# Who begins the weight loads of the first layer: SyncE or ScalarE

## The chip, the cores and the metric

The kernel runs on one core of a Trainium2 chip. The metric is the device time of one launch in microseconds (us), as the median of some runs. The core has five engines with a queue of instructions each: TensorE (PE in the rows; PEld is its weight load), VectorE (DVE), ScalarE (ACT), GpSimd (POOL) and SyncE (SP). SyncE computes nothing and only begins transfers. The transfers themselves are carried out by 16 DMA engines, whichever engine began them. Engines wait for one another through semaphores.

## What is computed

The reference, cut to what matters (4 batches, 8 heads, 576 queries and keys, head size 64; then two dense blocks over 2304 tokens, 512 features wide with 2048 hidden features):

```python
def _attn_ref(q, k, v, tau):
    scale = 1.0 / np.sqrt(q.shape[-1])
    scores = scale * np.matmul(q, k.transpose(0, 1, 3, 2))
    thresh = np.max(scores, axis=-1, keepdims=True) - tau
    scores = np.where(scores >= thresh, scores, -1000000000.0)
    scores = scores - np.max(scores, axis=-1, keepdims=True)
    attn = np.exp(scores)
    attn = attn / (np.sum(attn, axis=-1, keepdims=True) + 1e-09)
    return np.matmul(attn, v)
# x = the heads side by side, (2304, 512)
# first layer:  g = s * relu(x @ w_in)**2 + b;   x = g @ w_out
# second layer: h = x @ w_in2;  g = h * sigmoid(1.702 * h);  out = g @ w_out2
```

## The kernel before

**Beats.** Attention is cut into 160 score tiles of up to 128 queries, two to a *beat*; there are 85 beats. The tiles belong to 32 groups of one pair of heads: *long* groups (384 queries, three beats) and *short* ones (192 queries, two beats). In each beat TensorE makes two tiles of scores, VectorE takes their row extremes (L1045) and masks them (L1071), ScalarE takes the exponent between the two (L1269), GpSimd norms the rows (L1554), and VectorE turns the tile in blocks of 32x32 into `blocks` (L1085), which has room for two groups.

**The moves.** The turned blocks still lie in the wrong partitions. SyncE puts them in place with transfers `prob_t <- blocks` (`move_quad`, L639 to L651, four transfers each). For a long group eight of them come in one beat (its first half) and eight in the next (its second half); for a short one eight and four. They wait until the whole group is turned and until the earlier readers of that half of `prob_t` are done. Two things wait for them: `context_of` on TensorE (L777 to L809), which multiplies `prob_t` with the values, and VectorE's first turn of the group after next (L1081 to L1084), which writes over `blocks`.

**The first layer beside it.** From beat 15 (`MLP_FROM`) on, each beat also holds one *step* s = beat - 15 of the first layer: one slab of 128 hidden features for a tile of 384 tokens. There are 96 steps; steps 0 to 69 run beside attention (beats 15 to 84), steps 70 to 95 alone. TensorE computes `hidden(s)` (L831) and `output(s - 3)` (L850); ScalarE makes the gate (L1325), the high part of the gated values (L1332), and the high parts of both weight slabs (`slab_in_hi` L1311, `slab_out_hi` L1318); GpSimd makes the low parts of the weights (L1560, L1567), in place, in the memory of `w_raw`. Each float32 product is made of three products of high and low parts.

**The loads.** Load n (512 KB) brings the input slab n and the output slab n - 3 from HBM into slot n mod 5 of `w_raw`. There are 99 loads (0 to 98); the first three and the last three carry only one of the two slabs. Load n waits until `hidden(n - 5)` and, from n = 8, `output(n - 8)` are done, since these read the slot. Loads 0 to 3 are begun by SyncE in beat 1; from beat 15 on SyncE begins load beat - 11, that is, s + 4, in each beat, and loads 74 to 98 in the steps after attention (L713 to L715).

**SyncE's order in a beat** is written by hand and never overtaken: loads of queries, loads of keys, the moves of that beat, the weight load (L687, L688), loads of values (L678 to L694). **ScalarE's order in a beat** (L1425 to L1461): exponents, copies of attention results, `gated_hi(s - 1)`, `slab_out_hi(s - 1)`, splits of queries and keys (L1253, L1259), `gate_of(s)`, `slab_in_hi(s + 2)`. In the beats in which a token tile ends, `gate_of` comes before `slab_out_hi`.

Of the kernel before, what the change touches and what calls it, by code (L numbers as in the profile page):

```python
# [118 lines left out]
def q_load_beat(i):  # L119
    return max(0, q_split_beat(i) - (1 if Q_LOADS[i][0] < LONE_GROUPS else 2))  # L120
# [38 lines left out]
def key_load_beat(e):  # L159
    return max(0, key_free_beat(e), key_split_beat(e) - 2)  # L160
# [15 lines left out]
STEPS = LAYER_TILES * SLABS  # L176
# [4 lines left out]
IN_HI, OUT_HI, LO_RING = 3, 3, 5  # L181
IN_LEAD = 3
# [49 lines left out]
MLP_FROM = 15  # L232
# [34 lines left out]
def riding(beat):  # L267
    return PIECE_OF[beat] if beat in PIECE_OF and rides(PIECE_OF[beat]) else None


def alone(beat):
    return PIECE_OF[beat] if beat in PIECE_OF and not rides(PIECE_OF[beat]) else None
# [42 lines left out]
def tiles_of(beat, lag=0):  # L315
    return range(2 * beat - lag, 2 * beat - lag + 2)
# [41 lines left out]
def build(nc, q, k, v, consts_in, ident_in, slabs, twin_in, twin_out, out):  # L358
    ctx = ExitStack()
    with ctx:  # L360
        def sem(name):
            return ctx.enter_context(nc.semaphore(name))

        def sbuf(stack, name, shape, dt=F32):
            return stack.enter_context(nc.sbuf_tensor(name, shape, dt))
# [48 lines left out]
        w_raw = sbuf(raw, "w_raw", [P, LO_RING, 2, D_MODEL])  # L414
# [83 lines left out]
        w_loaded = [sem(f"w_loaded{n}") for n in range(LO_RING)]  # L498
# [4 lines left out]
        h_ready = sem("h_ready")  # L503
# [4 lines left out]
        y_step_done = sem("y_step_done")  # L508
# [39 lines left out]
        def out_of(ring, n):  # L548

            return ring[:, (n + IN_LEAD) % LO_RING, 1, :]  # L550
# [10 lines left out]
        def h_bank(n):  # L561

            if n < FIRST_PURE:
                return shared
            return (scores[0][:, 1, :], scores[1][:, 0, :], scores[1][:, 1, :])[n % H_RING]
# [50 lines left out]
        def _(sp):  # L616
            def load_q(i):

                if i >= Q_RING:
                    sp.wait_ge(q_lo_ready, i - Q_RING + 1)  # L620
                sp.dma_start(q_raw[:, i % Q_RING, 0:q_width(i)], q[i][:, 0:q_width(i)]).then_inc(q_loaded[i % Q_RING], 16)

            def load_k(e):

                if key_slot(e) >= STORE and key_before(e) is None:
                    sp.wait_ge(context_ready, LONE_PIECES)
                if key_before(e) is not None:
                    sp.wait_ge(scores_ready, key_tiles(key_before(e))[-1] + 1)
                if e >= 2:
                    sp.wait_ge(k_hi_ready, e - 1)  # L630
                sp.dma_start(k_raw[key_slot(e)][:], k[e]).then_inc(k_loaded[e % 2], 16)

            def load_values(i):

                if i >= 2:
                    sp.wait_ge(context_ready, VALUES[i - 2][2] + 1)
                sp.dma_start(v_sb[:, i % 2, :, :, :], v[i]).then_inc(v_loaded[i % 2], 16)
# [15 lines left out]
            def move_quads(w, beat):  # L653
                for a in range(quads_of(w)):
                    if beat == FIRST_BEAT[w] + (4 if is_long(w) else 3) + a // 2:
                        move_quad(w, a)

            def load_weights(n):

                parts = slice(0 if n < STEPS else 1, 1 if n < IN_LEAD else 2)  # L660
                if n >= LO_RING:
                    sp.wait_ge(h_ready, n - LO_RING + 1)
                if n >= LO_RING + IN_LEAD:
                    sp.wait_ge(y_step_done, n - LO_RING - IN_LEAD + 1)
                sp.dma_start(w_raw[:, n % LO_RING, parts, :], slabs[slab_row(n), :, parts, :]
                             ).then_inc(w_loaded[n % LO_RING], 16)
# [11 lines left out]
            for beat in range(BEATS):  # L678
                for i in range(3, len(Q_LOADS)):
                    if q_load_beat(i) == beat:  # L680
                        load_q(i)
                for e in range(2, HEADS):
                    if key_load_beat(e) == beat:
                        load_k(e)
                for w in range(PE_GROUPS, len(GROUPS_OF)):
                    move_quads(w, beat)
                if beat >= MLP_FROM:  # L687
                    load_weights(beat - MLP_FROM + IN_LEAD + 1)  # L688
                if beat == 1:
                    for n in range(IN_LEAD + 1):  # L690
                        load_weights(n)
                for i in range(2, len(VALUES)):
                    if PIECES[VALUES[i - 2][2]][2] == beat:
                        load_values(i)  # L694
# [549 lines left out]
        def _(act_eng):  # L1244
# [16 lines left out]
            def exponent(j):  # L1261

                m, r = rows_of(j), j % STATS
                act_eng.wait_ge(max_ready, j + 1)
                if PROBS <= j < PE_TILES + PROBS:
                    act_eng.wait_ge(rows_pe_turned, j - PROBS + 1)
                elif j >= PROBS:
                    act_eng.wait_ge(turned, j - PROBS - PE_TILES + 1)
                nc.scalar.activation(prob[0:m, j % PROBS, :].rearrange("p (a n) -> p a n", a=2),  # L1269
                                     scores[j % 2][0:m, :, 0:HALF], ACT.Exp,  # L1270
                                     bias=neg_max[0:m, r:r + 1], scale=-1.0).then_inc(exp_ready, 1)

            def context_hi(piece):

                c, start = piece_place(piece)
                act_eng.wait_ge(context_ready, piece + 1)
                if start >= HALF_TOKENS and piece_place(piece - 1)[1] < HALF_TOKENS:
                    act_eng.wait_ge(scores_ready, key_tiles(2 * HEADS_PER_BATCH - 1)[-1] + 1)
                nc.scalar.copy(act_at(act_hi, c, start, piece_size(piece)), piece_bank(piece)
                               ).then_inc(context_hi_ready, 1)  # L1280
# [32 lines left out]
            def slab_out_hi(n):  # L1313

                act_eng.wait_ge(w_loaded[(n + IN_LEAD) % LO_RING], 16 * ((n + IN_LEAD) // LO_RING + 1))
                if n >= OUT_HI:
                    act_eng.wait_ge(y_step_done, n - OUT_HI + 1)
                nc.scalar.copy(wout_hi[n % OUT_HI][:], out_of(w_raw, n)).then_inc(wout_hi_ready, 1)  # L1318

            def gate_of(n):  # L1320

                act_eng.wait_ge(h_ready, n + 1)
                if n >= 2:
                    act_eng.wait_ge(g_lo_ready, n - 1)
                nc.scalar.activation(gate[:, n % 2, :], h_bank(n)[:, 0:TOK], ACT.Relu).then_inc(gate_ready, 1)  # L1325
# [90 lines left out]
            def tile_ends(s):  # L1416
                return s >= OUT_LAG and (s - OUT_LAG) % SLABS == SLABS - 1
# [7 lines left out]
            for beat in range(BEATS):  # L1425
                s = beat - MLP_FROM
                if alone(beat - 1) is not None:
                    context_hi(alone(beat - 1))
                for j in tiles_of(beat):
                    if j < TILES:  # L1430
                        exponent(j)
                    if j % 2 == 0 and 0 <= j - 4 < PE_TILES:
                        copy_tails(j - 4)
                    if j % 2 == 0 and turn_due(s) is not None:
                        x_riding(s)
                if riding(beat) is not None:
                    context_hi(riding(beat))
                for j in tiles_of(beat, 4):
                    if 0 <= j < PE_TILES:
                        copy_main(j)  # L1440
                if tile_ends(s - 1) and s + 1 < STEPS:
                    slab_in_hi(s + 1)
                if s >= 1:
                    gated_hi(s - 1)
                if tile_ends(s):
                    copy_rows(s - OUT_LAG)
                    if s < STEPS:
                        gate_of(s)
                if s >= 1:
                    slab_out_hi(s - 1)  # L1450
                for i in range(2, len(Q_LOADS)):
                    if q_split_beat(i) == beat:
                        split_q(i)
                for e in range(2, HEADS):
                    if key_split_beat(e) == beat:
                        split_k(e)
                if not tile_ends(s):
                    if 0 <= s < STEPS:
                        gate_of(s)
                    if 0 <= s + 2 < STEPS:  # L1460
                        slab_in_hi(s + 2)  # L1461
# [181 lines left out]
def slab_row(n):  # L1643
    return n % SLABS
# [57 lines left out]
```

## Time and profile before

| | us |
|---|---|
| median of 3 runs | 1011.58 (1011.28 to 1013.16) |
| the profiled execution | 1009.4 |
| its span from first to last instruction | 1007.6 |

| engine | busy, us | share of the span |
|---|---|---|
| TensorE, matmul | 993.2 | 99% |
| TensorE, weight load | 895.4 | 89% |
| VectorE | 798.0 | 79% |
| GpSimd | 657.9 | 65% |
| ScalarE | 606.6 | 60% |

The granted TensorE clock is at its full level in all 40 slices of the span. All of the kernel's own transfers stand on one DMA queue, "q1 hardware_dynamic", with 141.34 MB. Times in the trace count from the span's start. Attention ends at about 490 us, the first layer at about 615 us; the rest is the second layer. In the rows, "PE L807" is an instruction of line 807 on TensorE, and "[0.86 <-DMA prob_t<-blocks]" is idle time of the engine just before the instruction, with what ended it. SyncE's instructions ("SPq") are the beginnings of transfers; their duration is the time that the beginning takes on SyncE's queue, and the landing of the data is told apart.

### The profile page before, as it was taken

To read this page: it belongs to the slowest core of one execution; us is meant where nothing else is said; L and a number is where in the kernel's file an instruction comes from. 1 tells how busy PE (TensorE), PEld (TensorE's weight loads), DVE (VectorE), ACT (ScalarE), POOL (GpSimd) and SP (SyncE) were. 2 spreads that over 40 slices of the span, in tenths; PEclk is the share of its full clock that TensorE was granted. 3 is DMA by queue.
4 is the path that set the end of the run, shared out by engine and by line. 5 is a ranking of instruction groups with operands and counts; after the bars stand their busy time and mean duration, and the time that the engine had idled before them with its cause. 6 is when DMAs were issued, how large, how long until landed. Compare 5 with 4: busy or idle time off the path is not lost.

```text
span 1007.6 us, 18212 instructions
## 1 busy us (share of the span) xinstructions
PE 993.2 (99%) x5922; PEld 895.4 (89%) x5922; DVE 798.0 (79%) x1749; ACT 606.6 (60%) x1124; POOL 657.9 (65%) x713
## 2 busy tenths in 40 slices
PE   8999999999999999999999999999999999999998
PEld 7788888888888888888899999998989989899897
DVE  7989999999999999999547766877767776566663
ACT  7877666666676666765555755555546555454443
POOL 6769997778788888886657775454544545445452
PEclk9999999999999999999999999999999999999999
DMA  7236776897977797778733541112122221222212
GB/s 216 73 116 187 209 204 189 218 239 213 228 199 191 204 246 190 209 179 217 211 106 126 185 150 32 63 42 85 44 82 87 102 84 46 81 87 102 84 48 79
DMA packets 97581, 142.50 MB, mean 141 GB/s; under 512 B 10320, under 2 KB 68944, under 8 KB 97488
## 3 DMA queue, kind: packets, MB, share of 16 engines
q1 hardware_dynamic: 97488, 141.34, 48.7%
q8 instruction: 49, 0.80, 0.3%
q14 instruction: 44, 0.36, 0.1%
HBM read 102.96 MB, written 4.72 MB: 107 GB/s over the span
## 4 chain that ended last, share of the span: by engine, by line
PE 85%; DVE 11%; issue 1%; DMA 1%; ACT 1%; POOL 0%; SPq 0%; DVEq 0%; POOLq 0%; ACTq 0%
PE shared L831 12%; PE y_ps L850 11%; PE shared L924 10%; PE y_ps L948 10%; PE scores L948 10%; PE scores L924 8%; PE scores L745 7%; PE scores L807 7%; PE scores L831 5%; PE y_ps L870 5%; DVE scores L1045 4%; DVE prob L1071 3%; PE scores L870 2%; DVE blocks L1085 1%; DMA k_raw<-k 1%
## 5 line engine op out<-in xcount | busy, mean ns | idle before, releaser
L1269 ACT ACTIVATE prob<-scores,neg_max 128x576 f32<-128x576 f32 (+1 forms) x160 | 118.6, 742 | 122.5 <-DVE scores L1045 122.4
L1614 POOL TENSOR_TENSOR a_sum_lo<-a_sum,a_hi 128x256 fp32r<-128x256 f32 x96 | 70.1, 740 | 182.5 <-DVE scores L1167 123.9
L1560 POOL TENSOR_TENSOR w_lo<-w_raw,win_hi 128x512 fp32r<-128x512 f32 x96 | 129.1, 1345 | 22.1 <-ACT win_hi L1311 17.7
L1567 POOL TENSOR_TENSOR w_lo<-w_raw,wout_hi 128x512 fp32r<-128x512 f32 x96 | 126.5, 1318 | 23.4 <-ACT wout_hi L1318 23.4
L1045 DVE TENSOR_SCALAR_CACHE_REDUCE scores<-scores,consts 128x576 f32<-128x576 f32 (+1 forms) x160 | 129.5, 809 | 13.1 <-PE scores L745 11.7
L1554 POOL TENSOR_SCALAR prob<-prob,row_inv 128x576 f32<-128x576 f32 (+1 forms) x160 | 126.8, 805 | 6.1 <-DVE row_inv L1059 5.7
L1071 DVE SCALAR_TENSOR_TENSOR prob<-scores,limit,prob 128x576 f32<-128x576 f32 (+1 forms) x160 | 128.1, 808 | 0.3
L831 PE MATMUL shared<-act_hi,win_hi 128*128 128x384 f32 x280 | 94.8, 339 | 1.1 <-DVE gate L1101 0.9
L831 PE MATMUL shared<-act_hi,w_lo 128*128 128x384 f32 x280 | 94.3, 337 | 0.0
L831 PE MATMUL shared<-act_lo,win_hi 128*128 128x384 f32 x280 | 93.9, 335 | 0.0
L1085 DVE STREAM_TRANSPOSE blocks<-prob 128x576 f32<-128x576 f32 (+1 forms) x128 | 91.4, 751 | 1.9 <-DMA prob_t<-blocks 1.7
L1108 DVE SCALAR_TENSOR_TENSOR g_lo<-gate,consts,g_hi 128x384 fp32r<-128x384 f32 x96 | 92.7, 966 | 0.2 <-ACT g_hi L1332 0.2
L1179 DVE TENSOR_TENSOR g_lo<-gate,g_hi 128x384 fp32r<-128x384 f32 x96 | 62.2, 650 | 33.4 <-ACT g_hi L1403 32.8
L745 PE MATMUL scores<-k_hi,q_hl 128*128 128x288 f32 (+1 forms) x320 | 76.6, 320 | 6.8 <-DVE prob L1071 6.2
L1332 ACT ACTIVATE g_hi<-gate,consts 128x384 fp32r<-128x384 f32 x96 | 59.0, 614 | 38.8 <-PE y_ps L870 27.9
L1395 ACT ACTIVATE gate<-scores 128x384 f32<-128x384 f32 x48 | 23.6, 492 | 94.9 <-DVE scores L1167 94.9
L1403 ACT CAST g_hi<-gate 128x384 fp32r<-128x384 f32 x96 | 49.2, 514 | 49.4 <-DVE gate L1174 40.0
L850 PE MATMUL y_ps<-wout_hi,g_hi 128*128 128x512 f32 x192 | 75.6, 394 | 0.0
L850 PE MATMUL y_ps<-wout_hi,g_lo 128*128 128x512 f32 x192 | 75.5, 393 | 0.0
L807 PE MATMUL scores<-prob_t,v_sb 128*64 128x192 f32 x800 | 73.8, 331 | 1.5 <-DVE prob L1071 0.9
L850 PE MATMUL y_ps<-w_lo,g_hi 128*128 128x512 f32 x192 | 74.9, 390 | 0.0
L1532 POOL TENSOR_TENSOR q_hl<-q_raw,q_hl 128x384 fp32r<-128x384 f32 (+1 forms) x51 | 49.0, 961 | 37.7 <-DVE g_lo L1108 31.2
(157 smaller groups left out, 2956.6 us busy)
## 6 DMA issues: line engine op xcount, KB each, us to landing
w_raw<-slabs SPq DMA_DIRECT2D x93, 512.0 KB, 4.2
a_raw<-twin_in SPq DMA_DIRECT2D x24, 512.0 KB, 4.6
o_raw<-twin_out SPq DMA_DIRECT2D x24, 512.0 KB, 3.6
prob_t<-blocks SPq DMA_DIRECT2D x96, 120.0 KB, 2.8
k_raw<-k SPq DMA_DIRECT2D x32, 288.0 KB, 4.6
prob_t<-blocks SPq DMA_DIRECT2D x96, 96.0 KB, 2.9
v_sb<-v SPq DMA_DIRECT2D x26, 320.0 KB, 4.3
q_raw<-q SPq DMA_DIRECT2D x40, 192.0 KB, 4.4
```

The lines of the kernel that those rows point to most:

```text
L745: mm = nc.tensor.matmul(scores[j % 2][0:m, half, 0:HALF], q_hl[i % Q_RING][:, q0:q0 + m], part[key_slot(e)][:, half * HALF:(half + 1) * HALF],
L807: mm = nc.tensor.matmul(place, v_sb[:, i % 2, side, c, :], rows, start=(c == 0), stop=(c == KEY_CHUNKS - 1))
L831: mm = nc.tensor.matmul(bank[:, 0:TOK], wp[:, w], act_at(xp, c, tile * TOK, TOK), start=(c == 0 and k == 0), stop=(c == DC - 1 and k == 2))
L850: mm = nc.tensor.matmul(y_ps[g][:], gp[:, n % 2, toks], wp[:, :], start=(f == 0 and k == 0), stop=(f == SLABS - 1 and k == 2))
L924: mm = nc.tensor.matmul(twin_bank(x), wp, xp, start=(c == 0 and k == 0), stop=(c == 1 and k == 2))
L948: mm = nc.tensor.matmul(z_bank(tile, g), gp[:, i, toks], wp, start=(e == 0 and i < 2 and k == 0), stop=(e == TWIN_SLABS - 1 and i >= 2 and ...
L1045: nc.vector.tensor_scalar(place, place, scale_c[0:m, :], None, ALU.mult, ALU.min, accum_out=neg_max[0:m, j % STATS:j % STATS + 1]).then_in ...
L1071: nc.vector.scalar_tensor_tensor(out=p, in0=scores[j % 2][0:m, :, 0:HALF], scalar=limit[0:m, r:r + 1], in1=p, op0=ALU.is_le, op1=ALU.mult, ...
L1269: nc.scalar.activation(prob[0:m, j % PROBS, :].rearrange("p (a n) -> p a n", a=2), scores[j % 2][0:m, :, 0:HALF], ACT.Exp, bias=neg_max[0: ...
L1554: nc.gpsimd.tensor_scalar(prob[0:m, j % PROBS, :], prob[0:m, j % PROBS, :], row_inv[0:m, r:r + 1], 1.0, ALU.mult, ALU.mult).then_inc(norme ...
L1560: nc.gpsimd.tensor_tensor(in_of(w_lo, n), in_of(w_raw, n), win_hi[n % IN_HI][:].bitcast(F32), ALU.subtract).then_inc(win_lo_ready, 1)
L1567: nc.gpsimd.tensor_tensor(out_of(w_lo, n), out_of(w_raw, n), wout_hi[n % OUT_HI][:].bitcast(F32), ALU.subtract).then_inc(wout_lo_ready, 1)
```

## The change

ScalarE begins the weight loads 4 to 73 instead of SyncE. In beat 15 + s it begins load s + 4, right behind `slab_out_hi(s - 1)` and ahead of the splits of queries and keys (in beats in which a token tile ends, `gate_of(s)` is already done by then). The waits are the same two semaphores, now waited for on ScalarE's queue. Loads 0 to 3 and 74 to 98 stay with SyncE. Nothing else changes.

```diff
--- before.py
+++ after.py
@@ -684,8 +684,6 @@
                         load_k(e)
                 for w in range(PE_GROUPS, len(GROUPS_OF)):
                     move_quads(w, beat)
-                if beat >= MLP_FROM:
-                    load_weights(beat - MLP_FROM + IN_LEAD + 1)
                 if beat == 1:
                     for n in range(IN_LEAD + 1):
                         load_weights(n)
@@ -1317,6 +1315,16 @@
                     act_eng.wait_ge(y_step_done, n - OUT_HI + 1)
                 nc.scalar.copy(wout_hi[n % OUT_HI][:], out_of(w_raw, n)).then_inc(wout_hi_ready, 1)
 
+            def load_weights(n):
+
+                parts = slice(0 if n < STEPS else 1, 2)
+                if n >= LO_RING:
+                    act_eng.wait_ge(h_ready, n - LO_RING + 1)
+                if n >= LO_RING + IN_LEAD:
+                    act_eng.wait_ge(y_step_done, n - LO_RING - IN_LEAD + 1)
+                nc.scalar.dma_start(w_raw[:, n % LO_RING, parts, :], slabs[slab_row(n), :, parts, :]
+                                    ).then_inc(w_loaded[n % LO_RING], 16)
+
             def gate_of(n):
 
                 act_eng.wait_ge(h_ready, n + 1)
@@ -1448,6 +1456,8 @@
                         gate_of(s)
                 if s >= 1:
                     slab_out_hi(s - 1)
+                if s >= 0:
+                    load_weights(s + IN_LEAD + 1)
                 for i in range(2, len(Q_LOADS)):
                     if q_split_beat(i) == beat:
                         split_q(i)
```

## Rows read from the trace of the kernel before

**Rows 1.** Stretches: length; PE, PEld, DVE, ACT, POOL busy us; clock; DMA share; GB/s.
```profile
66.00:120.00 54.00, 51.63 (x331) 45.29 (x328) 51.45 (x133) 40.01 (x79) 49.97 (x54) 1.00 0.66 194
...
300.00:400.00 100.00, 99.91 (x644) 88.35 (x642) 96.08 (x240) 67.26 (x127) 83.02 (x93) 1.00 0.80 212
```

**Rows 2.** Chain that ended last: start, us, what; 255 to 270.
```profile
255.25 2.10 PE shared L831 x12
...
260.47 2.10 PE shared L831 x12
...
267.74 2.10 PE shared L831 x12
```

**Rows 3.** Timeline of SyncE's queue, 289 to 310: start, us, line, operation.
```profile
289.91 0.53 SPq L665 DMA_DIRECT2D w_raw<-slabs  x1
...
291.93 5.24 SPq L649 DMA_DIRECT2D prob_t<-blocks  x8
297.27 0.53 SPq L665 DMA_DIRECT2D w_raw<-slabs  x1
...
309.56 0.33 SPq L665 DMA_DIRECT2D w_raw<-slabs  x1
```

**Rows 4.** The same queue: one long weight-load issue, two second-half batches.
```profile
243.85 1.46 SPq L665 DMA_DIRECT2D w_raw<-slabs  x1
...
357.30 5.47 SPq L649 DMA_DIRECT2D prob_t<-blocks  x8
...
422.09 5.19 SPq L649 DMA_DIRECT2D prob_t<-blocks  x8
```

**Rows 5.** DMA view, issue to landing: moves at 289.3, 296.8, 362.4, 427.0; load at 297.3.
```profile
prob_t<-blocks SPq DMA_DIRECT2D x1, 96.0 KB, 2.3
...
prob_t<-blocks SPq DMA_DIRECT2D x1, 96.0 KB, 5.6
...
prob_t<-blocks SPq DMA_DIRECT2D x1, 96.0 KB, 4.9
...
prob_t<-blocks SPq DMA_DIRECT2D x1, 96.0 KB, 5.4
...
w_raw<-slabs SPq DMA_DIRECT2D x1, 512.0 KB, 6.9
```

**Rows 6.** Timeline: first readers of the moves on PE, and VectorE's wait.
```profile
165.09 0.51 PE L807 MATMUL scores<-prob_t,v_sb 128*64 128x192 f32 x3 [0.24 <-DMA prob_t<-blocks]
...
302.29 1.44 DVE L1085 STREAM_TRANSPOSE blocks<-prob 128x576 f32<-128x576 f32 x2 [0.86 <-DMA prob_t<-blocks]
...
302.79 0.54 PE L807 MATMUL scores<-prob_t,v_sb 128*64 128x192 f32 x3
...
367.79 0.38 PE L807 MATMUL scores<-prob_t,v_sb 128*64 128x192 f32 x2
...
433.22 0.55 PE L807 MATMUL scores<-prob_t,v_sb 128*64 128x192 f32 x4
```

**Rows 7.** Timeline of ACT and DVE around 295, and a slab's use.
```profile
294.63 0.60 ACT L1318 CAST wout_hi<-w_raw 128x512 fp32r<-128x512 f32 x1
...
295.66 0.47 ACT L1325 ACTIVATE gate<-shared 128x384 f32<-128x384 f32 x1
...
297.52 0.60 DVE L1101 SCALAR_TENSOR_TENSOR gate<-shared,consts,gate 128x384 f32<-128x384 f32 x1
...
310.02 0.61 ACT L1311 CAST win_hi<-w_raw 128x512 fp32r<-128x512 f32 x1
```

**Rows 8.** Timeline of ACT and DVE in beat 16.
```profile
77.51 0.62 ACT L1318 CAST wout_hi<-w_raw 128x512 fp32r<-128x512 f32 x1
78.02 0.51 ACT L1325 ACTIVATE gate<-shared 128x384 f32<-128x384 f32 x1
...
78.67 0.60 DVE L1101 SCALAR_TENSOR_TENSOR gate<-shared,consts,gate 128x384 f32<-128x384 f32 x1
```

**Rows 9.** One microsecond in which mostly loads ran (columns as in Rows 1).
```profile
358.00:359.00 1.00, 1.00 (x8) 1.00 (x7) 0.96 (x4) 0.69 (x2) 1.00 (x2) 1.00 1.00 400
```

## The prediction

> **What bounds the kernel now.** I read the stretches first. Between 300 and 400 us TensorE is busy for 99.91 of 100 us, with VectorE at 96.08 [rows 1]. A busy TensorE says little by itself, since its matmuls overlap, so I looked next at the rhythm in the chain of waits: the first-layer products begin at 255.25, 260.47 and 267.74, so a beat without a context product takes 5.22 us and one with it 7.27 us [rows 2]. These two lengths (7.15 to 7.27, and 0.2 us more where rows are transposed) come back in every beat from 34 to 78, and the chain there passes through TensorE alone. This is a floor that TensorE sets by its own work. The reader is to see that nothing which merely frees another engine can shorten these 45 beats. Only the first part has air: from 66 to 120 us TensorE is idle for 54 - 51.63 = 2.4 us, and VectorE is busy for 51.45 of these 54 [rows 1]; VectorE sets the pace there.
>
> Then I read SyncE's queue, since the change takes work from it. A weight load holds it for 0.53 us behind other transfers, 0.33 us where the queue was quiet [rows 3], and once 1.46 us [rows 4]. A second-half batch of eight moves takes 5.24 us to begin [rows 3]. The DMA view gives the time from beginning to landing: a move at the end of a first-half batch lands after 2.3 us, one at the end of the following second-half batch after 5.6 us [rows 5]. So by the second batch the DMA engines are behind: load 38, values, queries and keys were begun between 289.91 and 291.93 [rows 3] and their bytes still stand ahead of the moves.
>
> **Part 1: the loads themselves.** 70 of 99 loads change hands. Load 39 was begun at 297.27 and took 6.9 us to land, at 304.2 [rows 3, 5]; its first reader comes at 310.02 [rows 7], a margin of 5.8 us, and it is among the smallest of the 70 (the least is 5.5). ScalarE begins load 39 behind the copy at 294.63 [rows 7], 2.6 us earlier; where it comes later than SyncE did, it is by at most 6 us in beats whose margin is over 11. Both waits are already met at that point: the gated values that ScalarE copied just before need `hidden(s - 1)`, and the copy itself waited for `output(s - 4)`. Cost of this part: nothing, covered by those margins.
>
> **Part 2: ScalarE's queue.** 70 beginnings are added. The trace has none on ScalarE, so I bound one from both sides: 0 if it runs beside the copy of 0.60 us ahead of it [rows 7], 0.33 to 0.53 if it takes its time alone as on SyncE [rows 3], 1.46 at worst [rows 4]; below zero is excluded, since work is only added. Queued behind it are the splits, the gate, the next input slab and the next exponent. The nearest to be missed is the gate: at 295.66 + 0.47 = 296.13 it is ready, VectorE takes it at 297.52 [rows 7], so 1.4 us are free there; over the beats from 18 on this slack is 1.1 us or more. An ordinary beginning costs nothing in those beats. In beat 16 it is different: the gate is ready at 78.02 + 0.51 = 78.53 and VectorE starts on it at 78.67 [rows 8], 0.14 us later, in the stretch where VectorE sets the pace. With 0.33 us on the queue, 0.33 - 0.14 = 0.2 us are lost and not won back. I take 0.2 (between 0 and 1.3), by the row of the quiet queue, since SyncE begins nothing else near 78.
>
> The Trainium skill, Perfetto Trace Analysis, "Per-engine timelines", says that a ScalarE instruction is pushed into a wait queue and the sequencer goes on to the next one; a beginning would then run beside the copy and the 0.2 would be 0. No run here shows a transfer begun by ScalarE.
>
> **Part 3: SyncE's queue.** Each beat loses about 0.58 us there (297.27 to the next beginning). What stood behind a load comes that much earlier: values, the next beat's queries, keys and moves. Where does anyone wait for them? TensorE waits once, 0.24 us at 165.09 [rows 6], for the short batch of group 11, which stood right behind a load. Gain: 0.24 us at most, and I take it. VectorE waits three times (the longest 0.86 us, at 302.29 [rows 6]) and the beats around keep their floor length, so that is worth nothing.
>
> **Part 4: the DMA engines.** This is the part that decides. Until now each load stood behind the batch of moves of its beat, in one queue. ScalarE begins it at its copy, and in the beats that end long groups this falls into the second-half batch: load 39 at about 295, into the batch of 291.93 to 297.17 [rows 3, 7]. The moves behind it then share the engines with 512 KB. In a microsecond full of loads they moved 400 GB/s, which is 0.4 MB in a us [rows 9], so the load's 0.512 MB are worth 1.28 us of all engines. The last moves of the batch land later by d. If the engines have no gap, d = 1.28; if the batch, begun 0.58 us earlier, keeps that lead, d = 0.7; if the two queues fill gaps of each other, d = 0, or below it by the 0.58; if the long packets of a load are taken before several short ones of a move, d could reach 2. I take 1.28, by the landing rows: 5.6 against 2.3 us [rows 5] say that the engines are behind, and an earlier beginning buys nothing then.
>
> How late may they be? The last of eight begins at 291.93 + 7/8 x 5.24 = 296.5 and lands at 302.1 (VectorE, waiting for it, starts at 302.29); TensorE's context product starts at 302.79: margin 0.7 us [rows 3, 5, 6]. The same sum at 357.30 gives 362.1 + 4.9 = 367.0 against 367.79, margin 0.8; at 422.09 it gives 426.6 + 5.4 = 432.0 against 433.22, margin 1.2 [rows 4, 5, 6]. There are six such places (second halves of groups 16 to 26, the even ones); the other three have 1.3, 1.4 and 1.6. All other batches have over 2.5 us. TensorE has no slack in these beats, so what goes past a margin lengthens the span. At d = 1.28 this is 0.58 + 0.48 + 0.08 = 1.14 us.
>
> Of the way in which the DMA engines choose between two queues nothing can be seen here, as only one queue is used. The Trainium skill, DMA: Bandwidth & Descriptors, "Queues, rings and completion order", says that each engine takes turns between the queues it has work for, packet by packet; load 39 would then not wait for the moves begun before it, which is the case with d above 0.7. The same page, "Issuing engines are not separate DMA queues", adds that a second issuing engine saves only time on the sequencer.
>
> **The sum.** +1.14 (part 4) + 0.2 (part 2) - 0.24 (part 3) = +1.1 us. The profiled execution would go from 1009.4 to 1010.5 (span 1007.6 to 1008.7). The median of the runs lies 2.2 us above the profiled execution, so the forecast is 1011.58 + 1.1 = 1012.7 us. A measurement of this kernel can tell about 0.2%, 2.0 us, from no change.
>
> **The rivals.** *All is hidden* (d below 0.7): the two queues fill each other's gaps. For it: in the heaviest microseconds the rate is well below 400 GB/s with moves alone. Time: 1011.58 + 0.2 - 0.24 = 1011.5. *The moves come too late* (slower): one mechanism, its place the six second-half batches. From d = 1.45 on the sum of what passes the six margins is over 1.9 us; at d = 2 it is 1.3 + 1.2 + 0.8 + 0.7 + 0.6 + 0.4 = 5.0, so 1016.6. For it: DMA share at or near 1 in that stretch [rows 9] and moves of small packets. Against it: 512 KB are worth only 1.28 at the rate seen. *ScalarE is held* (slower): while SyncE begins eight moves, ScalarE's beginning takes 1.46 us or more, and passes the gate's slack of 1.1 by 0.36. VectorE, at 96%, wins back little of that. In some 12 beats with a batch in the way this is 12 x 0.36 = 4.3, so 1015.9. *SyncE's relief is worth something* (faster): moves, queries and keys come 0.58 us earlier. Its ceiling is TensorE's idle time from 66 to 120 us, 2.4 us [rows 1], and the 0.24 at 165, if all of it hung on SyncE: 1011.6 - 2.6 = 1009.0; but most of these stalls are released by VectorE, not by transfers. That ScalarE begins its loads at a point far from SyncE's and nothing at all changes is part of the first rival.
>
> **Chances.** Forecast (d from 0.7 to 1.45, 1011.5 to 1013.5) 0.45; all hidden 0.17; moves too late 0.22; ScalarE held 0.08; faster by over 2 us 0.08. Hence faster 0.08, within 0.2% 0.62, slower 0.30. For 8 in 10 the range takes in the forecast, the hidden case and most of the slower ones: 1010.8 to 1016.6.
>
> **What would show it.** Part 2: a row of ScalarE's queue for each load, 0.3 to 0.6 us long, and idle time before VectorE's L1101 in beat 16. Part 3: no more wait before the context product near 165. Part 4: landing times of the last moves of the six batches up from 5.6, 4.9 and 5.4 by about 1.3; VectorE's wait at 302 grown from 0.86 towards 2; TensorE's L807 waiting for DMA at two or three places with 1.1 us in all; beats elsewhere still 5.2 and 7.2 us long. The prediction is wrong if the beats between the six places change length, if the landing times do not move, or if anything differs behind attention, where the change touches nothing.

## The result, and the profile after

The changed kernel takes 1012.31 us (median of 18 runs, 1010.30 to 1016.06), the kernel before on the same chip 1009.71 us (18 runs, 1008.58 to 1013.16). The ratio is 1.0026, 95% interval 1.0016 to 1.0037: it is 1.6 to 3.7 us slower, 2.6 us at the median. A second comparison on another occasion (below) gave 1.0012. I had forecast +1.1 us.

The page of the profile after (its span is 1012.2 us, 4.6 us above the 1007.6 us of before):

```profile
span 1012.2 us, 18212 instructions
...
q1 hardware_dynamic: 87408, 104.63, 38.2%
q10 hardware_dynamic: 10080, 36.70, 11.9%
...
PE 79%; DVE 10%; DMA 4%; SPq 4%; issue 2%; ACT 1%; POOL 0%; ACTq 0%; DVEq 0%
...
w_raw<-slabs ACTq DMA_DIRECT2D x70, 512.0 KB, 4.4
```

The 70 loads have gone to a queue of their own, q10, with 36.70 MB, and the chain that ended last now runs through DMA and SyncE's queue for 4% each (before: 1% and 0%). The waits from 66 to 500 us (engine, line, what it waited for: us in total, times, longest) say for what:

```profile
DVE blocks L1083 <- DMA prob_t<-blocks: 10.0, 6, 3.4
PE scores L805 <- DMA prob_t<-blocks: 4.5, 4, 2.2
```

Before, VectorE waited for moves three times [rows 6 has the longest, 0.86 us]; now six times, and TensorE's 4.5 us are nearly the whole growth of the span. These are TensorE's four waits in its timeline (start, length, line, and in brackets the idle time before it and what ended it):

```profile
271.01 1.85 PE L805 MATMUL scores<-prob_t,v_sb 128*64 128x192 f32 x20 [0.85 <-DMA prob_t<-blocks]
305.79 1.85 PE L805 MATMUL scores<-prob_t,v_sb 128*64 128x192 f32 x20 [2.22 <-DMA prob_t<-blocks]
371.96 1.85 PE L805 MATMUL scores<-prob_t,v_sb 128*64 128x192 f32 x20 [1.11 <-DMA prob_t<-blocks]
404.78 1.85 PE L805 MATMUL scores<-prob_t,v_sb 128*64 128x192 f32 x20 [0.34 <-DMA prob_t<-blocks]
```

and these are three of VectorE's six, in its timeline, the largest and the two where TensorE does not wait:

```profile
305.66 1.44 DVE L1083 STREAM_TRANSPOSE blocks<-prob 128x576 f32<-128x576 f32 x2 [3.43 <-DMA prob_t<-blocks]
338.05 1.44 DVE L1083 STREAM_TRANSPOSE blocks<-prob 128x576 f32<-128x576 f32 x2 [0.52 <-DMA prob_t<-blocks]
437.29 1.44 DVE L1083 STREAM_TRANSPOSE blocks<-prob 128x576 f32<-128x576 f32 x2 [0.80 <-DMA prob_t<-blocks]
```

The reader is to see that 271, 305, 338, 371, 404 and 437 are the second halves of groups 16, 18, 20, 22, 24 and 26: the six places of part 4, and no other. I call them the six batches, and the load of the same beat (steps 30, 35, 40, 45, 50 and 55) the load inside; the load of the step before it is the load ahead.

At 290 to 298 the queues of ScalarE and SyncE show how one of them comes about (start, length, line, transfer; compare [rows 3] and [rows 7]):

```profile
290.35 0.33 ACTq L1325 DMA_DIRECT2D w_raw<-slabs  x1
292.16 5.46 SPq L649 DMA_DIRECT2D prob_t<-blocks  x8
293.29 0.74 ACT L1267 ACTIVATE prob<-scores,neg_max 128x576 f32<-128x576 f32 x1 [0.88 <-DVE scores L1043]
293.59 0.34 ACTq L1325 DMA_DIRECT2D w_raw<-slabs  x1
293.93 0.61 ACT L1309 CAST win_hi<-w_raw 128x512 fp32r<-128x512 f32 x1
...
294.95 0.61 ACT L1316 CAST wout_hi<-w_raw 128x512 fp32r<-128x512 f32 x1
```

The load inside is begun at 293.59, while the exponent still runs and 1.36 us ahead of the copy that stands in front of it in the program. In most of the 70 beginnings, this one among them, the load comes about 0.3 us behind the end of TensorE's last product of `output(s - 4)`, for which it has to wait. What the engines then did, one microsecond each from 296, 297, 298 and 299 (DMA queue: packets, MB, time of its packets as a share of 16 engines):

```profile
q1 hardware_dynamic: 272, 0.24, 97.7%
q10 hardware_dynamic: 7, 0.03, 20.5%
...
q10 hardware_dynamic: 31, 0.13, 69.1%
q1 hardware_dynamic: 86, 0.06, 42.7%
...
q10 hardware_dynamic: 49, 0.20, 88.8%
q1 hardware_dynamic: 28, 0.02, 11.9%
...
q10 hardware_dynamic: 46, 0.14, 52.8%
q1 hardware_dynamic: 167, 0.12, 50.9%
```

In the two microseconds ahead of these, from 294 to 296, q10 moved nothing, so for some 2.5 us the load hardly moves a byte. (The load ahead, begun at 290.35, has no packet in q10 before 291 either, so a part of the 2.5 us comes with any load.) Then it has most of the engines for about three microseconds, and the moves in q1 fall from 0.24 MB in a microsecond to 0.02. With the two microseconds behind these (9.4% and 1.7%) q10's packets take 2.4 us of all 16 engines for 0.52 MB. The two moves begun last meanwhile landed late (issues within 296.9 to 297.65; size, median us from issue to landing):

```profile
prob_t<-blocks SPq DMA_DIRECT2D x2, 96.0 KB, 7.9
```

Before, the two begun last took 5.1 us. (For the very last move alone it is 8.5 us here, and 5.6 before [rows 5].)

### The profile page after: what moved, and what is told of

Same layout as the page of the kernel before. It is cut to its first block, busy times and chain, and to the rows that moved or that the text cites. A ratio compares the mean times of both kernels' runs of the same rounds, so it can differ in the third digit from the quotient of the medians.

```text
span 1012.2 us, 18212 instructions
## 1 busy us (share of the span) xinstructions
PE 993.5 (98%) x5922; PEld 896.0 (89%) x5922; DVE 797.7 (79%) x1749; ACT 607.7 (60%) x1124; POOL 658.5 (65%) x713
## 3 DMA queue, kind: packets, MB, share of 16 engines
q10 hardware_dynamic: 10080, 36.70, 11.9%
## 4 chain that ended last, share of the span: by engine, by line
PE 79%; DVE 10%; DMA 4%; SPq 4%; issue 2%; ACT 1%; POOL 0%; ACTq 0%; DVEq 0%
PE shared L922 10%; PE scores L946 10%; PE y_ps L946 10%; PE shared L829 10%; PE y_ps L848 9%; PE scores L922 8%; PE scores L805 6%; PE scores L743 6%; PE scores L829 5%; PE y_ps L868 5%; DVE scores L1043 4%; SPq L649 3%; DMA prob_t<-blocks 3%; DVE prob L1069 3%; PE scores L868 2%
```

## The experiments

Each was timed in 5 rounds beside the kernel before; the medians are of 11 runs where no other number is given. All start from the kernels before and after; `SIX = (30, 35, 40, 45, 50, 55)` are the steps of the loads inside.

**The change once more**, as a reference for the next three.

> The changed kernel itself again, for a second profile and as the yardstick of the other kernels of this group. Both theories: 2 to 4 us over the kernel before (ratio about 1.003); TensorE waits for moves three or four times before its context products (L805), 3 to 5 us in all; VectorE waits for moves about 10 us in all.

Measured: 1011.23 us against 1010.27, ratio 1.0012 (1.0004 to 1.0021). VectorE's waits for moves are 6.9 us, TensorE's 1.6. All three are less than I had expected of a mere repetition. The places are the same, only that group 16 has no wait this time; the size varies from one profiled execution to another (at group 18 VectorE waits 1.51 us here and 3.43 us above). The two comparisons overlap between 1.0016 and 1.0021.

**Six loads given back to SyncE**, behind their batch, the other 64 on ScalarE.

```diff
+                if beat - MLP_FROM in SIX:
+                    load_weights(beat - MLP_FROM + IN_LEAD + 1)
...
-                if s >= 0:
+                if s >= 0 and s not in SIX:
                     load_weights(s + IN_LEAD + 1)
```

> Six of the 70 loads (steps 30, 35, 40, 45, 50, 55, whose ScalarE beginning falls into the second-half batches of groups 16 to 26) are begun by SyncE again, behind the batch; the other 64 stay on ScalarE. Theory A (those six loads push their batch's last moves past the margin): all of the loss goes; ratio to the kernel before 1.000 (within 0.001), no wait of TensorE for moves before context products of those groups, last landing of the batches as before (about 10 us from the batch's first beginning). Theory B (a second queue beside the moves slows the engines everywhere, or SyncE's transfers crowd once it is relieved): most of the loss stays, ratio 1.002 or more.

Measured: 1009.23 us, ratio 0.9991 (0.9982 to 1.0000). No engine waits for a move between 66 and 500 us. The last moves of group 18's batch (issues 295.9 to 296.8) take 4.2 us instead of 7.9:

```profile
prob_t<-blocks SPq DMA_DIRECT2D x2, 96.0 KB, 4.2
```

So the loss hangs on six of the 70 loads. But 4.2 is also less than the 5.1 of before, though the load inside is where it was. Something else got better.

**Only those six on ScalarE**, 64 on SyncE as before.

```diff
+                if beat >= MLP_FROM and beat - MLP_FROM not in SIX:
+                    load_weights(beat - MLP_FROM + IN_LEAD + 1)
...
+                if s in SIX:
                     load_weights(s + IN_LEAD + 1)
```

> Only those six loads are begun by ScalarE; the other 64 stay with SyncE. Theory A: all of the loss is there, ratio about 1.003, TensorE's waits for moves 3 to 5 us as in the full change. Theory B: six loads are 9% of the change, so ratio under 1.001.

Measured: 1019.31 us (4 runs), ratio 1.0084 (1.0071 to 1.0097), three to seven times the loss of the whole change. This was expected by neither theory. Its waits:

```profile
DVE blocks L1088 <- DMA prob_t<-blocks: 16.1, 6, 4.5
PE scores L810 <- DMA prob_t<-blocks: 9.3, 5, 3.5
```

**All on SyncE, the six ahead of their batch** in its queue (the diff moves `load_weights` for `SIX` above `move_quads`, and ScalarE begins none).

> All loads on SyncE's one queue; the same six stand ahead of their batch of moves instead of behind it, so that their bytes are served first, without a second queue. Theory A1 (the bytes alone count, 1.28 us of all engines each, plus 0.58 us by which the batch is begun later): last moves later by 1.3 to 1.9 us, TensorE waits 1.2 to 3.5 us, ratio 1.001 to 1.003. Theory A2 (two queues side by side cost more than their bytes, as the 3 us by which the changed kernel's moves at 305 were late suggest): clearly less loss here than in the kernel with the six on ScalarE, each wait at most 1.2 us against up to 2.2.

Measured: 1018.86 us (6 runs), ratio 1.0090 (1.0073 to 1.0106), waits of 16.1 and 9.4 us:

```profile
DVE blocks L1090 <- DMA prob_t<-blocks: 16.1, 6, 4.5
PE scores L812 <- DMA prob_t<-blocks: 9.4, 6, 3.6
```

One queue or two, the sums of the waits are the same. Place by place they differ (at group 18 VectorE waits 3.26 us with two queues and 2.06 with one, at group 20 it is 1.79 and 3.00), and the load inside is begun 1.2 us earlier here, so this is no exact comparison; but a second queue is not needed for the loss. What counts is that 512 KB come before the last moves. The size was far above both of my expectations, and as large as in the run before. What those two runs have in common is the load ahead. Taking T as the start of the last transposition before the one that waits (327.86 to 360.44 and so on in before), the issue times at the six places are:

| kernel | load ahead | load inside | VectorE's waits | TensorE's waits | ratio |
|---|---|---|---|---|---|
| before | T - 5.2 | T + 2.2 | 1.7 | 0 | 1 |
| changed | T - 7.4 | T - 1.9 | 10.0 / 6.9 | 4.5 / 1.6 | 1.0026 / 1.0012 |
| six back | T - 7.4 | T + 2.3 | 0 | 0 | 0.9991 |
| six only | T - 5.3 | T - 1.9 | 16.1 | 9.3 | 1.0084 |
| six ahead | T - 5.2 | T - 3.1 | 16.1 | 9.4 | 1.0090 |

(Issue times are medians of the six places; waits are those for moves at the six, in us. At group 18 the changed kernel brings the load ahead only 0.4 us sooner, T - 5.6 against T - 5.2; at group 16 it is T - 7.4 against T - 6.6.) The rows at group 22 in "six only": the load ahead at 359.47 stands on SyncE behind a batch of moves, the load inside comes 2.9 us later, and VectorE waits 4.46 us.

```profile
359.47 0.54 SPq L668 DMA_DIRECT2D w_raw<-slabs  x1
362.40 0.35 ACTq L1330 DMA_DIRECT2D w_raw<-slabs  x1
362.80 6.11 SPq L652 DMA_DIRECT2D prob_t<-blocks  x8
375.56 1.44 DVE L1088 STREAM_TRANSPOSE blocks<-prob 128x576 f32<-128x576 f32 x2 [4.46 <-DMA prob_t<-blocks]
```

In the changed kernel these two are 5.6 us apart (355.99 and 361.57). New theory B: the change does two things to each batch. It brings the load ahead 2.2 us sooner, out of the batch's way, which is a gain, and puts the load inside before the last moves, which is a loss. The rival, C: what the whole change has in its favour is SyncE's relief in the other 58 beats.

**Twelve on ScalarE**, the six inside and the six ahead (as "only those six", with 29, 34, 39, 44, 49 and 54 in the list too).

> Twelve loads on ScalarE, 58 on SyncE: the six inside the batches and the six directly ahead of them (steps 29, 34, 39, 44, 49, 54). With the six alone on ScalarE the waits were 16.1 us on VectorE and 9.3 us on TensorE, and the ratio 1.0084, three times as bad as the whole change. In its trace the load ahead stood on SyncE 5.2 us before the last turn, 2.3 us later than in the changed kernel (7.4 us before it), so the two loads follow each other by 3.3 us instead of 5.5. Theory B (the load ahead is the reason: two loads' bytes come together before the last moves): with it moved too the waits fall to about those of the whole change, VectorE 6 to 10 us, TensorE 1.5 to 4.5 us, ratio 1.001 to 1.003. Rival C (SyncE's relief in all the other beats is what the whole change lives on): waits stay near 16 and 9 us, ratio 1.007 to 1.009.

Measured: 1012.82 us (8 runs), ratio 1.0028 (1.0017 to 1.0038), as the whole change.

```profile
DVE blocks L1088 <- DMA prob_t<-blocks: 7.7, 5, 2.8
PE scores L810 <- DMA prob_t<-blocks: 3.3, 3, 1.7
```

Theory B says 6 to 10 and 1.5 to 4.5, C says 16 and 9. B holds: six more loads moved take 6 us of TensorE's waiting away, and the other 58 do nothing that can be measured. It holds place by place too. VectorE's waits at groups 16 to 26 are 2.41, 3.26, 1.79, 4.46, 2.77 and 1.44 us in "six only" and none, 2.82, 0.72, 2.04, 1.67 and 0.45 here: at groups 20 to 26 the load ahead comes over 2 us sooner than in "six only" and the wait falls by 1.0 to 2.4 us; at group 18 it comes 0.2 us sooner and the wait falls by 0.4. Group 16 fits less well: 0.9 us sooner, and a wait of 2.4 us gone. Moving the load ahead also lets SyncE begin its batch 0.1 to 0.5 us sooner at the six places; no run separates this part from the load's own bytes.

**Only the six ahead on ScalarE**, the other 64 loads on SyncE. The edit is that of "only those six on ScalarE" with another list.

```diff
+SIX = (29, 34, 39, 44, 49, 54)
```

> The kernel before with only six loads on ScalarE, each the one directly ahead of a second-half batch (steps 29, 34, 39, 44, 49, 54); the load inside the batch stays on SyncE, behind it. Theory B (the load ahead adds its bytes to the same queue of work, and ScalarE brings it 2.3 us sooner and SyncE's batch 0.4 us sooner): VectorE's waits for moves fall from 1.7 us to under 0.3 us, no wait of TensorE at these places, ratio 0.9985 to 1.000, thus as good as with 64 loads on ScalarE. Rival C (the other 58 loads on ScalarE are what made the two best variants a little faster): waits of 1 us or more stay, ratio 1.000 to 1.001.

Measured: 1009.30 us against 1010.20, ratio 0.9987 (0.9978 to 0.9996). No wait for moves is left. This is the gain alone: it is the only variant whose interval lies wholly below 1 (though not by much), and six loads bring as much as 64.

**Half the bytes inside.** In the six beats ScalarE begins only the input half (256 KB), and SyncE brings the other half behind the batch.

```diff
+                if beat - MLP_FROM in SIX:
+                    n = beat - MLP_FROM + IN_LEAD + 1
...
+                    sp.dma_start(w_raw[:, n % LO_RING, 1:2, :], slabs[slab_row(n), :, 1:2, :]).then_inc(half_loaded, 16)
...
-                parts = slice(0 if n < STEPS else 1, 2)
+                parts = slice(0 if n < STEPS else 1, 1 if n - IN_LEAD - 1 in SIX else 2)
```

> The changed kernel, but at the six second-half batches (steps 30, 35, 40, 45, 50, 55) ScalarE begins only the input half of its load (256 KB) and SyncE brings the output half (256 KB) behind the batch, where the whole load stood before the change. The result is complete. Theory A (the bytes that go ahead of the last moves set the delay, the six loads being the cause): half the bytes, half the delay. In the change run again VectorE waited for moves 6.9 us in all and TensorE 1.6 us; above the margins little is left: VectorE 1 to 3 us, TensorE under 0.5 us, ratio 0.999 to 1.000. Rival Q (that anything at all stands on a second queue in these beats is what costs, not how much): the waits stay at 5 to 8 and 1 to 3 us, ratio 1.001 to 1.002.

Measured: 1009.75 us, ratio 0.9999 (0.9990 to 1.0008), as theory A has it. But the profiled execution showed 5.7 and 2.2 us of waits, which is the rival's number. It was the longest of eleven (1012.74 us), so I took it again.

> The variant with half the bytes inside the six batches once more. Its first profile was that of its slowest execution (1012.74 against a median of 1009.75) and showed waits for moves of 5.7 us on VectorE and 2.2 us on TensorE, 3.3 and 2.0 of them at one place. If the bytes set the delay, a profile near the median shows VectorE 1 to 4 us, TensorE under 1 us, and the ratio stays between 0.999 and 1.001. If anything at all inside the batch costs the same, the waits are again 5 us and 2 us or more, although the median does not show it.

Measured: 1009.82 us, ratio 0.9996 (0.9987 to 1.0005), and in this profile (span 1006.8 us) a single row of waits for moves:

```profile
DVE blocks L1092 <- DMA prob_t<-blocks: 1.2, 3, 0.4
```

Both medians say that with half the bytes nearly nothing is lost, so the amount of bytes counts. It isn't all that counts: in the first profile VectorE waited 3.26 us and TensorE 1.99 at group 18, as long as with the whole load (3.43 and 2.22), and in the second neither waited there, with load and batch begun at the same distance from T.

**The load held behind the copy.** All 70 on ScalarE, with a wait for the copy's own end, so that the order of the program becomes the order in time.

```diff
                if n >= LO_RING + IN_LEAD:
                    act_eng.wait_ge(y_step_done, n - LO_RING - IN_LEAD + 1)
+                if n > IN_LEAD + 1:
+                    act_eng.wait_ge(wout_hi_ready, n - IN_LEAD - 1)
```

> The changed kernel, with one more wait: ScalarE begins a load only when its copy of the output slab is done. In the trace of the changed kernel the load at the six places is begun 1.9 to 2.3 us ahead of VectorE's last turn of the first tile (0.3 at one of them) and the copy begins 1.0 us ahead of it, so this puts the load 1.6 to 2.0 us later, to about 0.35 us ahead of that turn, into the middle of the batch. If the prediction's sum failed because the load begins sooner than it assumed (the sequencer running ahead of the copy), the waits shrink: VectorE under 4 us in all, TensorE under 1 us, ratio 0.9995 to 1.0005. If the load's bytes take the place of the last moves wherever they come inside the batch, the waits stay within a factor of 1.5 of the change run again (VectorE 5 to 10 us, TensorE 1 to 4.5 us), ratio 1.001 to 1.003.

Measured: 1016.62 us (5 runs, 1014.60 to 1016.77), ratio 1.0058 (1.0046 to 1.0071). The waits are 8.4 and 3.4 us, in the second theory's range: a load 1.6 us later inside the batch does no less harm. This is not quite one change, since the hold also makes the load ahead about 1 us later (T - 6.3 for T - 7.4), and by theory B that costs too. The ratio is outside both. The profile shows two more costs. One is the queue (beat 16, ScalarE):

```profile
79.18 0.62 ACT L1319 CAST wout_hi<-w_raw 128x512 fp32r<-128x512 f32 x1
79.88 0.33 ACTq L1330 DMA_DIRECT2D w_raw<-slabs  x1
80.27 0.49 ACT L1338 ACTIVATE gate<-shared 128x384 f32<-128x384 f32 x1 [0.47 <-ACT wout_hi L1319]
```

The other is TensorE's clock (stretch: its length, PE busy, PEclk as the granted clock, DMA share, GB/s):

```profile
366.00:369.00 3.00, 3.00 (x16) 1.00 1.12 221
369.00:372.00 3.00, 1.44 (x10) 1.00 1.14 241
372.00:375.00 3.00, 2.39 (x18) 0.67 1.15 261
375.00:378.00 3.00, 3.00 (x17) 0.76 0.46 106
378.00:381.00 3.00, 3.00 (x18) 1.00 0.01 4
```

After a wait of 2.17 us for moves the granted clock is below full in the stretches from 372 to 378: 3 x (0.33 + 0.24) = 1.7 us of full clock are missing. From T = 362.84 to the next T at 398.98 are 36.14 us, against 32.10 in "six back": 4.04 more, of which 2.17 are the wait; the other 1.87 go with the clock. Against "six back" this profile is already 1.4 us behind at 25 us, ahead of every load that the edit touches, so that part doesn't belong to it; what made it is open.

**The six held until the next beat.** All 70 on ScalarE, the six begun only when the next beat's exponent may start, at T + 4.0.

```diff
+                if s - 1 in SIX:
+                    act_eng.wait_ge(exp_ready, 2 * beat + 1)
+                    load_weights(s + IN_LEAD)
...
-                if s >= 0:
+                if s >= 0 and s not in SIX:
```

> The changed kernel, all 70 loads on ScalarE, but the six are held back until the next beat's exponent may start, by when SyncE has begun the whole batch. Theory A (bytes ahead of the last moves): the six delays are gone although the loads stay on the second queue; VectorE's waits for moves under 1 us, TensorE's 0, ratio 0.998 to 1.000, as with the six given back to SyncE. Rival Q (a second queue by itself slows the moves): waits of 4 us or more remain, ratio 1.001 or more.

Measured: 1009.24 us, ratio 0.9991 (0.9982 to 1.0000), one wait of VectorE of 0.2 us, none of TensorE. All loads on the second queue and no loss.

**The same, once more, and held behind the copy as well**, to price the held queue by itself.

> The variant with the six loads held until the next beat, once more, on the chip of the two others and as their reference. It should repeat: ratio 0.998 to 1.000, no wait of TensorE for moves, VectorE's under 1 us; and it should not differ from the variant with six loads ahead of the batches on ScalarE by more than 0.1%.

> As the variant with the six loads held until the next beat, but every load is also held behind ScalarE's own copy of its slab. No load stands inside a second-half batch, so the moves cost nothing and what is left is the price of holding ScalarE's queue. In the trace of the change held behind its copy the first-layer products of beat 16 to 17 are 5.22 us apart where they are 4.75 us apart in the variants without the hold, and nowhere else does a beat without a wait for moves grow. Theory: +0.5 us against the six-late variant of the same call, all of it at about 80 us: ratio 0.9993 to 1.0001. Rival (the hold costs in every beat, which the six places hid): +2 us or more, ratio 1.001 or above.

Measured: 1009.49 us, ratio 0.9992 (0.9983 to 1.0001), without the hold; 1009.96 us, ratio 1.0000 (0.9991 to 1.0009), with it. TensorE waits for no move in either; VectorE does with the hold, twice, 1.0 us in all. The difference of 0.47 us is what beat 16 shows. In TensorE's timeline the first products of beats 15 and 16 without the hold are these:

```profile
74.28 0.42 PE L832 MATMUL shared<-act_hi,win_hi 128*128 128x384 f32 x1
79.03 0.41 PE L832 MATMUL shared<-act_hi,win_hi 128*128 128x384 f32 x1 [0.53 <-DVE gate L1102]
```

and with it these:

```profile
74.85 0.42 PE L832 MATMUL shared<-act_hi,win_hi 128*128 128x384 f32 x1
80.08 0.41 PE L832 MATMUL shared<-act_hi,win_hi 128*128 128x384 f32 x1 [1.01 <-DVE gate L1102]
```

4.75 us from product to product become 5.23, and TensorE's wait for VectorE's gate grows from 0.53 to 1.01. The intervals of the two overlap, so the timed difference alone would not show it; the rows do.

## Why the prediction was right, and where it was not

The time was inside the range (1010.8 to 1016.6) and the sign of the forecast was right. That 1012.31 lies so close to the forecast 1012.7 is luck: I had added 1.1 us to 1011.58, the median of three runs, and with 18 runs the kernel before is at 1009.71, 1.9 us lower. What can be compared is the difference: +1.1 forecast, +2.6 and +1.2 measured. By the bound of 0.2% the first comparison (0.26%) lies just over it, among the slower cases I gave 0.30, and the second (0.12%) within it, where I had put 0.62. It would be too much to say that one of these is settled.

**Part 1, the loads themselves: right.** No engine waits for a weight load in any profile, also where six come 6 us later than the change has them.

**Part 2, ScalarE's queue: the size was wrong, 0.2 against 0.** I set a beginning between the copy and the gate, as the program has it. In the trace ScalarE begins the load beside its exponent, 0.33 us long, ahead of the copy; in beat 16 nothing moved. This is the case that the page Perfetto Trace Analysis of the Trainium skill, "Per-engine timelines", describes (a ScalarE instruction goes into a wait queue, and the sequencer goes on to the next), and the trace agrees: 0 was the right value. What I had computed is the price of the held queue. It exists, in just the beat where I looked for it, and is 0.48 us: held, the gate starts 80.27 - 79.18 = 1.09 us behind the copy's start, where it starts 0.51 us behind it in before [rows 8]. That is 0.58 us later; less the slack of 0.14 it is 0.44, near the 0.48.

**Part 3, SyncE's relief: half right.** TensorE's wait near 165 [rows 6] is gone, as forecast. The failed step is the sentence that VectorE's waits at 302 and two other places are worth nothing. It is true of those waits, but I stopped there: behind a load in SyncE's queue stands the next batch, and ahead of the last moves stand the load's bytes. Taken off SyncE, the load ahead comes 2.2 us sooner and the batch up to 0.5 us sooner. The experiments price this: without it the same load inside costs 8.5 us instead of 1.2 to 2.6. So it was worth 6 to 7 us, second only to the load inside itself, and hidden in a row that I had read only for its 0.58 us.

**Part 4, the DMA engines: the right six places, the right mechanism, a wrong size.** The forecast was d = 1.28 and 1.14 us in all at three of them; TensorE waited at four with 4.5 us in the first profile and at three with 1.6 in the second. By the two moves begun last, d at group 18 was 7.9 - 5.1 = 2.8 us in the first and 6.3 - 5.1 = 1.2 in the second. Neither is the price of the bytes, because two terms of opposite sign stand in them. Against the same kernel with the load inside taken away (4.2 us) the moves land 3.7 and 2.1 us later: that is the load inside. The load ahead, and the earlier batch, give back 5.1 - 4.2 = 0.9 us. All six places say the same, with the last landing counted from T: "six back" is 0.9 to 2.0 us earlier than before (mean 1.4), the changed kernel 0.4 to 2.6 later in the first profile (mean 1.6) and from 0.1 earlier to 1.8 later in the second (mean 0.95). So the load inside costs 3.0 and 2.4 us on average, the earlier load and batch give back 1.4, and my 1.28 lies between the two net means without either term being right. The mis-sized step is 0.512 MB (0.52 in the trace) by 400 GB/s [rows 9]: that microsecond held mostly loads, all in q1. Inside the batch q10 moved 0.20 MB with 88.8% of the engines, that is 0.23 MB per microsecond of all engines, and the load took 2.4 us of them. With 2.4 for 1.28, and 0.9 given back, a net 1.5 comes out at group 18, between the two measured. That the forecast of the total came near is partly luck: one term too small and one missing, of opposite sign. TensorE had a cushion, as the margins say: its waits are VectorE's less 0.9 to 1.2 us (1.79 and 0.85, 3.43 and 2.22, 2.03 and 1.11, 1.47 and 0.34), and at 338 and 437, where VectorE's are 0.52 and 0.80, it does not wait.

**The rivals.** "All is hidden" falls: six rows of waits. "Moves too late", with d from 1.45 on, is what the profile after shows at four places (groups 16, 18, 22 and 24, with d from 1.6 to 2.6 counted from T) and the second profile at two (at d = 1.45 the rounded margins give 1.85 us, not over 1.9); its 5.0 us were nearly reached in that profile (4.6) and not in the medians. "ScalarE is held" needs a hold that the change does not make; with one made, it cost 0.48 us in one beat and not 4.3 in twelve. "SyncE's relief is worth something" was right in kind but in another place: not from 66 to 120 us, where nothing changed (TensorE busy 51.63 us before, 51.65 after), but ahead of the six batches, and it is seen only when the load inside does not eat it. The variants that keep it (six back, six late, and only the six loads ahead on ScalarE) are at 0.9987 to 0.9992, some 1 us below the kernel before. That they gain by removing occasional waits of before at the same places is inferred: before's profile has 1.7 us of VectorE's waits and none of TensorE at the six places. The spread of the runs fits it: the variant with only the six loads ahead on ScalarE ran from 1008.98 to 1009.76 us and the kernel before, timed beside it, from 1009.26 to 1013.47, so the low ends are 0.3 us apart and the high ones 3.7.

**What stays open.** Why the same program shows 3.43 us at group 18 in one execution and 1.51 in another. The issue times of load and batch, counted from T, differ by 0.5 us at most there. With half the bytes the same place shows 3.26 us and nothing, and there the issue times agree. And why the load stands still for 2.5 us and is then served nearly alone, which may decide whether moves behind it or beside it suffer; no run here varies this.

## What to carry to other kernels

When a transfer is moved to another engine's queue, write down for every batch that has a deadline which bytes are begun before its last transfer, with the load in front of the moved one too; only the six of 70 loads inside such a batch mattered, and the six in front of them mattered as much. A transfer that an engine begins is not tied to the compute instruction above it; it starts when its own semaphores allow, and if that is inside a critical batch, hold it by a semaphore that fires behind the batch, not by the neighbouring instruction. Take the rate for such a sum from the stretch where it collides, not from the best microsecond.

## What the runs showed of the hardware that I had not expected

**TensorE's granted clock fell after some single waits of 2 to 4 us.** In "six ahead" it happened twice (columns as above):

```profile
336.00:339.00 3.00, 1.56 (x10) 1.00 1.02 196
339.00:342.00 3.00, 2.54 (x17) 0.59 0.73 225
342.00:345.00 3.00, 3.00 (x17) 0.84 0.69 181
...
375.00:378.00 3.00, 1.17 (x10) 0.85 0.78 163
378.00:381.00 3.00, 3.00 (x19) 0.58 0.93 250
```

0.58 is near the lower of its two levels, 1.2 of 2.4 GHz, for most of the stretch. Both follow waits for moves, of 1.90 and 3.59 us. In "six only" a wait of 3.53 us at the same place left the clock at 1.00, so the wait does not decide alone. With equal waits (9.3 and 9.4 us) the spans of these two profiles are 1017.4 and 1020.4: 3.0 us for two such drops, 1.5 each. The distances from T to T say nearly the same: those that hold the two waits are 36.21 and 37.40 us, where "six back" has 32.59 and 32.10; less the waits this leaves 1.7 us each. A late transfer can thus cost more than the wait it causes.

**The two queues did not share evenly.** In the microsecond from 298 q10 had 88.8% and q1 11.9% of the engines, and from 295, over a microsecond after the load was begun, q10 had none and q1 79.0%. The page DMA: Bandwidth & Descriptors of the Trainium skill, "Queues, rings and completion order", lets each engine take turns packet by packet between the queues it has work for; over microseconds this trace shows blocks instead of an even mix. Whether both queues had packets ready in each of these microseconds the trace doesn't show: from 295 the engines were not even full, so the load's late start may be no matter of turns at all. The same page says under "Issuing engines are not separate DMA queues" that transfers begun by several engines run on the same 16 DMA engines and that only time on the sequencer is saved. The waits agree: in sum they were the same with one queue and with two (16.1 and 9.3 against 16.1 and 9.4 us).
